# A gated linear-attention recurrence with 64x64 array quarters for its rows, logits and scores

## The chip, the cores and the metric

One core of a Trainium2 chip runs the whole program. The metric is the device time of one execution in microseconds (us): the median of several executions of the same compiled program.

## The reference

The program is three stages in a row; the change touches the first alone. In code, cut to what matters:

```python
# q, k, v, f_logit: [4, 8, 768, 48] = batch, heads, sequence, head size
f = 1 / (1 + exp(-f_logit))
for t in range(768):
    state = f[:, :, t, :, None] * state + einsum('bhd,bhe->bhde', k[:, :, t], v[:, :, t])
    y[:, :, t] = einsum('bhd,bhde->bhe', q[:, :, t], state)
x = y as 3072 rows of 384
logits = (x / |x|) @ (emb / |emb|).T / tau      # 8 experts
out = gate * (relu(x @ w1[e]) @ w2[e])          # e = the best expert of the row
a = out @ m1; b = out @ m2; result = ((a * b) @ w3) @ w_out
```

## The kernel before, in words

The recurrence is computed in 24 tiles of 128 time steps (6 chunks of 4 batches; all 8 heads in each tile). The products of a tile on TensorE are, in the order in which one step s issues them (`step` of the tensor block):

- `scores(s)`: for each head, keys times queries, 48 (stored as 64) rows of contraction, 128x128 out, into the banks `b_a0` and `b_a1`. VectorE's `mask(s)` multiplies them by a triangle and puts them into `am`.
- `cumulate(s+2)`: a triangle of ones times the logarithms of the decay, in two parts (`lg_hi`, `lg_lo`), into `b_cum`. VectorE's `bound` takes the smaller of the sums and 60 into `cc`; ScalarE's `exps` makes exp(-cc) into `ec` and exp(cc) into `en`; GpSimd's `scale_q` multiplies the queries by `ec`, VectorE's `scale_k` the keys by `en`.
- `rows_and_logits(s-1)`: turns the finished y of the tile before (copied by ScalarE's `copy_yT` to `yT`, features on partitions) into rows with time on partitions, by products with `pick`, an identity beside the expert embeddings, into the bank `b_x`. VectorE's `take_rows` copies the rows to `x_ring` and sums the logits over the head pairs.
- `turn_qk(s+1)`: transposes of the scaled queries and keys into `b_qT` and `b_kT`, copied by ScalarE (`copy_qT`) and VectorE (`copy_kT`).
- `state_products(s)`: the carried state times the queries, 64x48 weights, into y's banks `b_y0` and `b_y1`.
- `chunk_products(s)`: values times the masked scores, added to the same banks; then y is done.
- `update_products(s)`: keys times values into `b_up`, a part of y's second bank. VectorE's `carry` adds the state, GpSimd's `decay` multiplies by the last decay of the tile, which goes through DRAM (`save_last`, `load_last` on the SP queue).

Each operation on float32 weights stands as two loads and two matmuls in the trace. Every engine runs its own `step` for s = -3 to 24; what sets the order is this written order on each engine, the semaphores between them and rings of four buffers for the loads. Steps 5 to 20 are a loop; in it ScalarE (`high_w3`, `high_wo`), VectorE (`low_wo`) and GpSimd (`low_w3`) also split two weight matrices into high and low parts, which stage three needs. After the last tile TensorE goes on with products of those weights (`w34_product`) while the rows are sorted by expert, and the two feed-forward stages follow.

An array "quarter" is a weight block on rows 0 to 63 or 64 to 127 and columns 0 to 63 or 64 to 127 of TensorE. Which one an instruction uses follows from the partitions of its operands (rows) and of its output (columns).

Of the kernel before, what the change touches and what calls it, by code (L numbers as in the profile page):

```python
# [27 lines left out]
P = 128  # L28
# [4 lines left out]
HP = 64  # L33
CH = S // P
# [24 lines left out]
CEIL = 60.0  # L59
# [53 lines left out]
def build(nc, ctx, qkvf, emb, tau, sets1, sets2, w3_t, w_out, out):  # L113
# [58 lines left out]
    cc = early("cc", [P, DM])  # L172
# [13 lines left out]
    pick = early("pick", [P, NP, 2 * D + E])  # L186
# [43 lines left out]
    SL = [pick[0:1].rearrange("p j n -> p (j n)")[:, k * (SLOTS + 2) * E:(k + 1) * (SLOTS + 2) * E].rearrange(  # L230
# [44 lines left out]
    YB = NP // 2 * P  # L275
    b_up = b_y1[:, YB:YB + NP * D]
# [4 lines left out]

    def y_place(j, g):

        if j < NP // 2:
            return b_y0[g * HP:g * HP + D, j * P:(j + 1) * P]
        return b_y1[(1 - g) * HP:(1 - g) * HP + D, (j - NP // 2) * P:(j - NP // 2 + 1) * P]
# [21 lines left out]
    clamp_done, ef_done, lg_done, ll_done, cum_done, bound_done, ec_done, exp_done = (sem(n) for n in (  # L308
        "clamp_done", "ef_done", "lg_done", "ll_done", "cum_done", "bound_done", "ec_done",
        "exp_done"))  # L310
# [33 lines left out]
    def _(sp):  # L344
# [60 lines left out]
        sp.wait_ge(pick_done, 1)  # L405
        for h in range(H):
            place = (h % 2 if h // 2 < NP // 2 else 1 - h % 2) * HP
            sp.dma_start(pick[place:place + D, h // 2, 2 * D:],
                         emb[:, h * D:(h + 1) * D].rearrange("e d -> d e"), allow_slow_non_contiguous=True
                         ).then_inc(emb_in, 16)  # L410
# [118 lines left out]
    def _(pool):  # L529
# [88 lines left out]
        pool.wait_ge(clamp_done, 2)  # L618
        pool.memset(ec[:, :, :, D:], 1.0)
# [53 lines left out]
    def _(pe):  # L673
        pe.wait_ge(masks_done, 3)

        def warm(n):

            for _ in range(n):
                pe.transpose(b_x[:, 0:P], ident[:], ident[:])

        def cumulate(i, r):

            pe.wait_ge(ll_done, i + 1)
            need(pe, bound_done, i)
# [18 lines left out]
        def state_products(i, r):  # L703
            for j in (0, NP // 2, 1, NP // 2 + 1):
                for g in range(2):
                    mm = pe.matmul(y_place(j, g), state[g * HP:(g + 1) * HP, r % 4, j, :],  # L706
                                   qT[g * HP:(g + 1) * HP, r % 2, j, :], start=(j % (NP // 2) == 0), stop=False,
                                   skip_group_check=True)
            mm.then_inc(sp_done, 1)

        def update_products(i, r):

            pe.wait_ge(ks_done, i + 1)
# [7 lines left out]
        def chunk_products(i, r):  # L721
            pe.wait_ge(am_done, i + 1)
            pe.wait_ge(v_landed[r % 4], (i - r % 4) * 4 + 16)
            for j in range(NP):
                for g in range(2):
                    h = 2 * j + g
                    mm = pe.matmul(y_place(j, g), ring_v[:, r % 4, h * D:(h + 1) * D],  # L727
                                   am[:, g, j, :], start=False, stop=True, skip_group_check=True)
# [13 lines left out]
        def rows_and_logits(i):  # L742

            pe.wait_ge(yT_done, i + 1)
            need(pe, rl_done, i)
            for j in range(NP):
                mm = pe.matmul(b_x[:, j * (2 * D + E):(j + 1) * (2 * D + E)], yT[:, j * P:(j + 1) * P], pick[:, j, :],  # L747
                               start=True, stop=True)
            if isinstance(i, int) and i == NORM_AT:
                pe.wait_ge(ones_done, 1)  # L750
                pe.wait_ge(en_sq_done, 1)
                mm = pe.matmul(b_x[:, NP * (2 * D + E):NP * (2 * D + 2 * E)], ones[:],
# [860 lines left out]
```

## Time and profile before

| | us |
|---|---|
| median of 3 runs | 716.99 |
| lowest, highest | 716.39, 717.34 |
| the profiled execution | 716.52 |
| its span | 714.6 |
| TensorE busy | 705.7 |
| VectorE, ScalarE, GpSimd busy | 339.8, 292.8, 193.2 |
| granted TensorE clock | 1.0 |

The span runs from the first to the last instruction. The recurrence takes about its first 143 us; the rest is the sorting and the two feed-forward stages. Busy shares are means over all stages, so the stage that is changed has to be read by itself: its timeline, the order of the operations on each engine, and what each waited for.

### The profile page before, as it was taken

The page shows a single profiled execution, that of the slowest core. Times are in us where ns is not written, and L with a number is a line of the kernel's source. Part 1 is how long each engine was busy: PE and PEld are TensorE (multiplying, and loading weights), DVE is VectorE, ACT ScalarE, POOL GpSimd, SP SyncE. Part 2 cuts the span into 40 slices and gives each one's busy share as a digit, 9 for nine tenths or more (in the row PEclk, how much of TensorE's full clock was granted, in tenths as well). Part 3 has the DMA queues.
Part 4 walks back from the last instruction along what each step waited for, and adds up shares of the span by engine and source line. Part 5 has one row for each costly group of instructions (what it writes and reads, how often), then busy time and mean ns, then how long its engine had stood idle before and what let it go on. Part 6 is the DMA issues. An engine that isn't in the chain of part 4 may idle for free.

```text
span 714.6 us, 13946 instructions
## 1 busy us (share of the span) xinstructions
PE 705.7 (99%) x4863; PEld 643.7 (90%) x4863; DVE 339.8 (48%) x564; ACT 292.8 (41%) x559; POOL 193.2 (27%) x197
## 2 busy tenths in 40 slices
PE   7999999999999999999999999999999999999997
PEld 6988888899999999999999988988989989889887
DVE  6888899678753545536556441312212112112121
ACT  5788888534443444435445342123022022121220
POOL 4567777202412022000000013034042051150242
PEclk9999999999999999999999999999999999999999
DMA  7788886261854443524244220000000010000001
GB/s 219 210 234 246 247 247 188 59 188 45 253 150 129 131 132 113 154 85 133 89 132 129 91 89 1 1 22 23 0 33 11 0 44 0 11 33 0 22 22 44
DMA packets 73056, 70.79 MB, mean 99 GB/s; under 512 B 20520, under 2 KB 61480, under 8 KB 73024
## 3 DMA queue, kind: packets, MB, share of 16 engines
q1 hardware_dynamic: 69952, 60.95, 28.9%
q0 software_dynamic: 3072, 9.44, 4.1%
q8 instruction: 17, 0.28, 0.2%
q14 instruction: 15, 0.12, 0.0%
HBM read 60.88 MB, written 9.49 MB: 98 GB/s over the span
## 4 chain that ended last, share of the span: by engine, by line
PE 94%; DVE 2%; issue 1%; DMA 1%; POOL 1%; ACT 1%; POOLq 0%; ACTq 0%; DVEq 0%; SPq 0%
PE b_a L768 10%; PE b_a L770 10%; PE b_a L769 10%; PE bank L768 9%; PE bank L770 9%; PE bank L769 9%; PE b_y L768 6%; PE b_y L769 6%; PE b_y L770 6%; PE b_a L694 4%; PE b_y L727 3%; PE bank L747 3%; PE bank L738 3%; PE b_y L706 2%; PE b_y L717 1%; PE bank L685 1%
## 5 line engine op out<-in xcount | busy, mean ns | idle before, releaser
L653 POOL TENSOR_TENSOR p_lo<-prod,p_hi 128x512 fp32r<-128x512 f32 x42 | 53.9, 1284 | 333.3 <-ACT p_hi L1154 333.3
L1151 ACT COPY a_sb<-b_a 128x512 f32<-128x512 f32 x48 | 28.2, 587 | 218.2 <-PE bank L770 218.2
L1562 DVE TENSOR_TENSOR prod<-bank,a_sb 128x512 f32<-128x512 f32 x48 | 33.2, 692 | 165.7 <-ACT a_sb L1151 165.7
L1104 ACT ACTIVATE h_hi<-b_a 128x432 fp32r<-128x432 f32 x64 | 34.0, 532 | 124.3 <-PE b_a L770 124.0
L1518 DVE SCALAR_TENSOR_TENSOR h_lo<-b_a,h_hi 128x432 fp32r<-128x432 f32 x64 | 38.8, 607 | 96.0 <-ACT h_hi L1104 96.0
L1179 DVE TENSOR_TENSOR w_lo<-w_raw,w_hi 128x768 fp32r<-128x768 f32 x72 | 67.9, 956 | 5.3 <-ACT w_hi L1067 1.2
L770 PE MATMUL b_a<-x_hi,w_lo 128*128 128x432 f32 x192 | 68.7, 358 | 0.0
L769 PE MATMUL b_a<-x_lo,w_hi 128*128 128x432 f32 x192 | 68.7, 358 | 0.0
L768 PE MATMUL b_a<-x_hi,w_hi 128*128 128x432 f32 x192 | 68.7, 358 | 0.0
L1067 ACT CAST w_hi<-w_raw 128x768 fp32r<-128x768 f32 x72 | 58.5, 833 | 0.0
L768 PE MATMUL b_a<-m_hi,w_hi 128*128 128x512 f32 x144 | 56.1, 390 | 0.6 <-DVE w_lo L1179 0.6
L769 PE MATMUL b_a<-m_lo,w_hi 128*128 128x512 f32 x144 | 56.1, 390 | 0.0
L770 PE MATMUL b_a<-m_hi,w_lo 128*128 128x512 f32 x144 | 56.1, 390 | 0.0
L768 PE MATMUL bank<-m_hi,w_hi 128*128 128x512 f32 x144 | 56.0, 389 | 0.0
L769 PE MATMUL bank<-m_lo,w_hi 128*128 128x512 f32 x144 | 56.0, 389 | 0.0
L770 PE MATMUL bank<-m_hi,w_lo 128*128 128x512 f32 x144 | 56.0, 389 | 0.0
L627 POOL DMA_INDIRECT xs<-x_recurrence,ids x24 | 25.9, 1080 | 110.4 <-PE bank L862 76.3
L768 PE MATMUL b_y<-h_hi,w_hi 128*128 128x432 f32 x128 | 46.9, 367 | 0.2
L769 PE MATMUL b_y<-h_lo,w_hi 128*128 128x432 f32 x128 | 45.7, 357 | 0.0
L770 PE MATMUL b_y<-h_hi,w_lo 128*128 128x432 f32 x128 | 45.7, 357 | 0.0
L768 PEld LDWEIGHTS b_a<-x_hi,w_hi 128*128 128x128 f32 x192 | 36.1, 188 | 1.5
L770 PEld LDWEIGHTS b_a<-x_hi,w_lo 128*128 128x128 f32 x192 | 36.1, 188 | 1.4
(247 smaller groups left out, 1626.1 us busy)
## 6 DMA issues: line engine op xcount, KB each, us to landing
w_raw<-sets SPq DMA_DIRECT2D x80, 192.0 KB, 3.5
w_raw<-sets SPq DMA_DIRECT2D x40, 384.0 KB, 4.0
ring_all<-qkvf SPq DMA_DIRECT2D x24, 384.0 KB, 3.8
ring_fc<-qkvf SPq DMA_DIRECT2D x24, 192.0 KB, 3.7
ring_all<-qkvf SPq DMA_DIRECT2D x24, 192.0 KB, 3.0
x_recurrence<-x_all SPq DMA_DIRECT2D x24, 192.0 KB, 3.6
w_sb<-w_t SPq DMA_DIRECT2D x8, 512.0 KB, 4.6
wo_sb<-w_out SPq DMA_DIRECT2D x8, 192.0 KB, 4.2
```

Source lines behind the costliest of these rows:

```text
L627: pool.indirect_dma_start(out=xs[:, w % BATCH, :], out_offset=None, in_=rec_dram.rearrange("b c p n -> (b c p) n"), in_offset=bass.Indirec ...
L653: pool.tensor_tensor(p_lo[:, f, :], prod[:, f % 2, :], p_hi[:, f, :].bitcast(F32), ALU.subtract).then_inc(pl_done, 1)
L694: mm = pe.matmul([b_a0, b_a1][g][:, j * P:(j + 1) * P], kT[g * HP:(g + 1) * HP, r % 2, j, :], qT[g * HP:(g + 1) * HP, r % 2, j, :], start= ...
L768: pe.matmul(acc, a_hi, b_hi, start=first, stop=False, skip_group_check=skip)
L769: pe.matmul(acc, a_hi, b_lo, start=False, stop=False, skip_group_check=skip)
L770: return pe.matmul(acc, a_lo, b_hi, start=False, stop=last, skip_group_check=skip)
L1067: act.copy(piece(w_hi, f), piece(w_raw, f)).then_inc(wh_done, 1)
L1104: act.activation(h_hi[:, f % 2, 0:SW], b_h[f % 2][:, 0:SW], ACT.Relu).then_inc(hh_done, 1)
L1151: act.copy(a_sb[:, f % 2, :], b_a[f % 2][:]).then_inc(as_done, 1)
L1179: return dve.tensor_tensor(out_, whole, high.bitcast(F32), ALU.subtract)
L1518: dve.scalar_tensor_tensor(out=h_lo[:, f % 2, 0:SW], in0=b_h[f % 2][:, 0:SW], scalar=0.0, in1=h_hi[:, f % 2, 0:SW].bitcast(F32), op0=ALU.m ...
L1562: dve.tensor_tensor(prod[:, f % 2, :], b_b[f % 2][:], a_sb[:, f % 2, :], ALU.mult).then_inc(pr_done, 1)
```

## The change

- Scores: each 64x128 weight block becomes two 64x64 blocks, so 16 products in place of 8, in the order in which four neighbours use the four quarters.
- Rows and logits: `yT` is laid out so that heads 0 to 3 stand on partitions 0 to 47 and heads 4 to 7 on 64 to 111 (`y_place`). The 4 products of 128x128 weights with 104 columns become 16 products of 48x64 weights with 56 columns, in quarters. They go to the inner halves of y's two banks (`b_rows`).
- The update gets `b_x`, the bank that rows had; `copy_yT` no longer waits for `carry` to have read it.
- `bound` is taken out. `exps` reads `b_cum` itself, and `scale_k` takes the smaller of `en` and exp(60) in the same instruction that multiplies the keys.
- Order on TensorE: `rows_and_logits` directly behind `scores`, then `cumulate`. On VectorE: `take_rows` ahead of `mask`; `mask` in two instructions, and `chunk_products` waits for each half; `low_logs` always behind `copy_kT`. On ScalarE: `copy_yT` ahead of `high_w3`.
- New waits: `state_products` waits for `rl_done` (VectorE has read the rows out of y's banks). `quarter()` issues an increment of a semaphore that nobody waits for, three times per tile on TensorE's queue. `exps(0)` waits for the padding of `ec`, which GpSimd writes later than before.
- At the start a memset of `yT` and two of four copies for `pick` go; the numbers of filling matmuls change from 14, 0, 10 to 16, 0, 4.

```diff
+    NS = NP // 2
+    y_parts = y_all.rearrange("p (a n) -> p a n", n=YB)[:, 0:4:3, :]
+    b_rows = y_all[:, 512 - NP * (D + E):512 + NP * (D + E)].rearrange("p (k n) -> p k n", n=D + E)
+    b_up = b_x[:, 0:NP * D]
     def y_place(j, g):
+        c = j // NS
+        return b_y01[c * HP:c * HP + D, g, g * YB + j % NS * P:g * YB + (j % NS + 1) * P]
...
+        def quarter():
+            pe.sem_inc(quarters, 1)
         def cumulate(i, r):
             pe.wait_ge(ll_done, i + 1)
-            need(pe, bound_done, i)
+            need(pe, exp_done, i)
         def scores(i, r):
             pe.wait_ge(qT_done, i + 1)
             pe.wait_ge(kT_done, i + 1)
-            need(pe, am_done, i)
+            need(pe, am_done, 2 * i)
+            quarter()
             for j in range(NP):
                 for g in range(2):
-                    mm = pe.matmul([b_a0, b_a1][g][:, j * P:(j + 1) * P], kT[g * HP:(g + 1) * HP, r % 2, j, :],
-                                   qT[g * HP:(g + 1) * HP, r % 2, j, :], start=True, stop=True)
+                    for c in range(2):
+                        mm = pe.matmul([b_a0, b_a1][g][c * HP:(c + 1) * HP, j * P:(j + 1) * P],
+                                       kT[g * HP:(g + 1) * HP, r % 2, j, c * HP:(c + 1) * HP],
+                                       qT[g * HP:(g + 1) * HP, r % 2, j, :], start=True, stop=True)
-        def state_ready(i):
-            need(pe, yT_done, i)
-            need(pe, sum_done, min(i, NT - B) if isinstance(i, int) else i)
-            need(pe, s_done, i - B + 1)
         def state_products(i, r):
+            need(pe, s_done, i - B + 1)
+            need(pe, rl_done, i)
+            quarter()
         def update_products(i, r):
-            pe.wait_ge(ks_done, i + 1)
+            need(pe, sum_done, min(i, NT - B) if isinstance(i, int) else i)
         def chunk_products(i, r):
-            pe.wait_ge(am_done, i + 1)
             pe.wait_ge(v_landed[r % 4], (i - r % 4) * 4 + 16)
+            for j in range(NS):
+                pe.wait_ge(am_done, 2 * i + (j + 1))
         def rows_and_logits(i):
             pe.wait_ge(yT_done, i + 1)
-            need(pe, rl_done, i)
-            for j in range(NP):
-                mm = pe.matmul(b_x[:, j * (2 * D + E):(j + 1) * (2 * D + E)], yT[:, j * P:(j + 1) * P], pick[:, j, :],
-                               start=True, stop=True)
+            quarter()
+            for j in range(NS):
+                for g in range(2):
+                    for c in range(2):
+                        for t in range(2):
+                            cols = slice((g * NS + j) * P + t * HP, (g * NS + j) * P + (t + 1) * HP)
+                            mm = pe.matmul(b_rows[t * HP:(t + 1) * HP, c * NP + 2 * j + g, :],
+                                           yT[c * HP:c * HP + D, cols], pick[c * HP:c * HP + D, 2 * j + g, :],
+                                           start=True, stop=True)
...
         def exps(i, r):
-            act.wait_ge(bound_done, i + 1)
+            act.wait_ge(cum_done, i + 1)
+            if isinstance(i, int) and i == 0:
+                act.wait_ge(pads_done, 2)
         def copy_yT(i):
             act.wait_ge(y_done, i + 1)
-            if not isinstance(i, int) or i < NT - B:
-                act.wait_ge(sum_done, i + 1)
...
         def scale_k(i, r):
-            dve.tensor_tensor(ks[:, r % 2, :, 0:D], ring_qk[:, r % 4, DM:2 * DM].rearrange("p (h d) -> p h d", h=H),
-                              en[:, r % 2, :].rearrange("p (h d) -> p h d", h=H), ALU.mult).then_inc(ks_done, 1)
-        def bound(i):
-            dve.wait_ge(cum_done, i + 1)
-            need(dve, exp_done, i)
-            dve.tensor_scalar_min(cc[:], b_cum[:, 0:DM], CEIL).then_inc(bound_done, 1)
+            dve.scalar_tensor_tensor(out=ks[:, r % 2, :, 0:D], in0=en[:, r % 2, :].rearrange("p (h d) -> p h d", h=H),
+                                     scalar=TOP,
+                                     in1=ring_qk[:, r % 4, DM:2 * DM].rearrange("p (h d) -> p h d", h=H),
+                                     op0=ALU.min, op1=ALU.mult).then_inc(ks_done, 1)
         def mask(i):
+            for j in range(NS):
+                dve.tensor_tensor(am[:].rearrange("p g (c j) t -> p g c j t", c=2)[:, :, :, j, :],
+                                  b_a01.rearrange("p g (c j t) -> p g c j t", c=2, t=P)[:, :, :, j, :],
+                                  upto[:].unsqueeze(1).unsqueeze(1).to_broadcast([P, 2, 2, P]), ALU.mult
+                                  ).then_inc(am_done, 1)
```

## Rows read from the trace of the kernel before

**Rows 1.** Windows: busy us (x) of PE, PEld, DVE, ACT, POOL; clock; DMA share; GB/s.

```profile
71.00:82.00 11.00, 11.00 (x176) 9.77 (x169) 10.09 (x20) 9.53 (x23) 8.39 (x9) 1.00 0.87 255
```

**Rows 2.** TensorE's timeline over one tile: start, duration, operation, count.

```profile
24.84 1.03 PE L747 MATMUL bank<-pick,yT 128*128 128x104 f32 x8
25.71 0.60 PE L738 MATMUL bank<-ident,qs 128*128 128x128 f32 x4
...
26.67 0.65 PE L706 MATMUL b_y<-qT,state 64*48 64x128 f32 x16
27.26 1.08 PE L727 MATMUL b_y<-am,ring_all 128*48 128x128 f32 x16
28.17 0.62 PE L717 MATMUL b_y<-ring_all,ks 128*64 128x48 f32 x16
28.72 1.16 PE L694 MATMUL b_a<-qT,kT 64*128 64x128 f32 x16
29.81 0.45 PE L685 MATMUL bank<-lg_hi,upto_r 128*128 128x384 f32 x1
```

**Rows 3.** TensorE's timeline: the scores of tiles 1 and 20.

```profile
17.86 1.16 PE L694 MATMUL b_a<-qT,kT 64*128 64x128 f32 x16
...
122.04 1.16 PE L694 MATMUL b_a<-qT,kT 64*128 64x128 f32 x16
```

**Rows 4.** Duration of one matmul in ns (min/median/max), by source line.

```profile
L706 PE MATMUL b_y<-qT,state x31: 269/269/307, 87.1 to 93.0; 64*48 64x128 f32 x31
...
L717 PE MATMUL b_y<-ring_all,ks x16: 206/222/222, 88.6 to 89.0; 128*64 128x48 f32 x16
```

**Rows 5.** VectorE's timeline in one tile.

```profile
89.88 0.55 DVE L1194 TENSOR_TENSOR ks<-ring_all,en 128x384 f32<-128x384 f32 x1
90.37 1.23 DVE L1210 TENSOR_TENSOR am<-b_a,upto 128x1024 f32<-128x1024 f32 x1
91.51 0.55 DVE L1200 TENSOR_SCALAR cc<-bank 128x384 f32<-128x384 f32 x1
92.05 0.89 DVE L1184 TENSOR_TENSOR lg_lo<-lg,lg_hi 128x384 fp32r<-128x384 f32 x1
92.86 0.55 DVE L1229 COPY x_all<-bank 128x384 f32<-128x384 f32 x1
...
93.43 0.68 DVE L1205 COPY kT<-bank 128x512 f32<-128x512 f32 x1
```

**Rows 6.** ScalarE's timeline in the same tile, with the idle time in brackets.

```profile
88.90 0.62 ACT L1015 CAST w_hi<-w_sb  x1
90.03 0.59 ACT L1000 COPY yT<-b_y 128x512 f32<-128x512 f32 x1 [0.51 <-issue]
```

**Rows 7.** GpSimd's and SP's timeline in the same tile.

```profile
90.78 1.28 POOL L577 TENSOR_TENSOR w_lo<-w_sb,w_hi  x1 [1.30 <-DVE ks L1194]
92.01 0.51 POOL L567 TENSOR_TENSOR state<-s_sum,e_all 128x192 f32<-128x192 f32 x1
...
93.29 0.39 SPq L370 DMA_DIRECT2D e_all<-last_rows  x1
```

**Rows 8.** The page's DMA issues: count, KB each, median us to landing.

```profile
e_all<-last_rows SPq DMA_DIRECT2D x24, 2.0 KB, 2.5
```

**Rows 9.** ScalarE's copy of y in the tile of rows 2 (timeline).

```profile
23.84 0.59 ACT L1000 COPY yT<-b_y 128x512 f32<-128x512 f32 x1 [1.12 <-PE b_y L727]
```

**Rows 10.** TensorE's sequencer instructions behind it: ns each, first and last start.

```profile
L72 PEldq EVENT_SEMAPHORE  x2: 51/51/51, 24.5 to 24.6; - x2
...
L736 PEldq EVENT_SEMAPHORE  x1: 51/51/51, 24.7 to 24.7; - x1
```

**Rows 11.** The first exponentials of the program, on ScalarE (timeline).

```profile
7.85 0.52 ACT L984 ACTIVATE ec<-cc 128x384 f32<-128x384 f32 x1 [1.33 <-DVE cc L1200]
```

**Rows 12.** TensorE's timeline in the last tile: rows, then state products.

```profile
138.84 1.06 PE L747 MATMUL bank<-pick,yT 128*128 128x104 f32 x8
139.83 0.65 PE L706 MATMUL b_y<-qT,state 64*48 64x128 f32 x16
```

More of the change, by code:

```diff
@@ L58 @@
 FLOOR = -40.0
-CEIL = 60.0
+TOP = float(np.exp(60.0))
 LEAST = 39.0
@@ L185, in build @@
     x_tile = early("x_tile", [P, DM])
-    pick = early("pick", [P, NP, 2 * D + E])
+    pick_all = early("pick_all", [P, NP * (2 * D + E)])
+    pick = pick_all[:, 0:NP * (D + E)].rearrange("p (k n) -> p k n", k=NP)
     upto = early("upto", [P, P])
@@ L229, in build @@
         "p (v i) -> p v i", v=3)
-    SL = [pick[0:1].rearrange("p j n -> p (j n)")[:, k * (SLOTS + 2) * E:(k + 1) * (SLOTS + 2) * E].rearrange(
+    SL = [pick_all[0:1, k * (SLOTS + 2) * E:(k + 1) * (SLOTS + 2) * E].rearrange(
         "p (t e) -> p t e", e=E) for k in range(2)]
@@ L404, in _ @@
         load_v(RING - 1, RING - 1)
-        sp.wait_ge(pick_done, 1)
+        sp.wait_ge(pick_done, 2)
         for h in range(H):
-            place = (h % 2 if h // 2 < NP // 2 else 1 - h % 2) * HP
-            sp.dma_start(pick[place:place + D, h // 2, 2 * D:],
+            place = h // NP * HP
+            sp.dma_start(pick[place:place + D, h % NP, D:],
                          emb[:, h * D:(h + 1) * D].rearrange("e d -> d e"), allow_slow_non_contiguous=True
@@ L721, in chunk_products @@
         def chunk_products(i, r):
-            pe.wait_ge(am_done, i + 1)
             pe.wait_ge(v_landed[r % 4], (i - r % 4) * 4 + 16)
-            for j in range(NP):
+            for j in range(NS):
+                pe.wait_ge(am_done, 2 * i + (j + 1))
                 for g in range(2):
-                    h = 2 * j + g
-                    mm = pe.matmul(y_place(j, g), ring_v[:, r % 4, h * D:(h + 1) * D],
-                                   am[:, g, j, :], start=False, stop=True, skip_group_check=True)
+                    for n in (j, j + NS):
+                        h = 2 * n + g
+                        mm = pe.matmul(y_place(n, g), ring_v[:, r % 4, h * D:(h + 1) * D],
+                                       am[:, g, n, :], start=False, stop=True, skip_group_check=True)
             mm.then_inc(y_done, 1)
@@ L751, in rows_and_logits @@
                 pe.wait_ge(en_sq_done, 1)
-                mm = pe.matmul(b_x[:, NP * (2 * D + E):NP * (2 * D + 2 * E)], ones[:],
-                               en_sq[:].rearrange("p j e -> p (j e)"), start=True, stop=True)
+                mm = pe.matmul(b_norm, ones[:], en_sq[:].rearrange("p j e -> p (j e)"), start=True, stop=True)
             mm.then_inc(xl_at, 1)
@@ L786, in step @@
             if isinstance(s, int) and s < 0:
-                warm({-3: 14, -2: 0, -1: 10}[s])
+                warm({-3: 16, -2: 0, -1: 4}[s])
             if (i := tile_of(s, 0)) is not None:
                 scores(i, r)
-            if (i := tile_of(s, 2)) is not None:
-                cumulate(i, r + 2)
             if isinstance(s, int) and s == NT:
@@ L802, in step @@
                 rows_and_logits(i)
-            if (i := tile_of(s, 0)) is not None:
-                state_ready(i)
+            if (i := tile_of(s, 2)) is not None:
+                cumulate(i, r + 2)
             if (i := tile_of(s, 1)) is not None:
@@ L1017, in step @@
         def step(s, r, part=None):
+            if (i := tile_of(s, -1)) is not None:
+                copy_yT(i)
             if part:
                 high_w3(*part)
-            if (i := tile_of(s, -1)) is not None:
-                copy_yT(i)
             if (i := tile_of(s, 3, 2)) is not None:
@@ L1251, in step @@
                 scale_k(i, r + 1)
-            if (i := tile_of(s, 0)) is not None:
-                mask(i)
-            if (i := tile_of(s, 2)) is not None:
-                bound(i)
-            if early_logs(s) and (i := tile_of(s, 3, 1)) is not None:
-                low_logs(i, r + 3)
             if isinstance(s, int) and s == NT:
@@ L1261, in step @@
                 take_rows(i, (r + RING - 1) % RING)
+            if (i := tile_of(s, 0)) is not None:
+                mask(i)
             if isinstance(s, int) and s == -3:
@@ L1265, in step @@
                 dve.wait_ge(emb_in, 16 * H)
-                dve.tensor_tensor(en_sq[:], pick[:, :, 2 * D:], pick[:, :, 2 * D:], ALU.mult).then_inc(en_sq_done, 1)
+                dve.tensor_tensor(en_sq[:], pick[:, :, D:], pick[:, :, D:], ALU.mult).then_inc(en_sq_done, 1)
             if (i := tile_of(s, 1)) is not None:
                 copy_kT(i, r + 1)
-            if not early_logs(s) and (i := tile_of(s, 3, 1)) is not None:
+            if (i := tile_of(s, 3, 1)) is not None:
                 low_logs(i, r + 3)
```

77 lines of the change are left out of this document (30 added, 47 removed).

## The prediction

> **What bounds the kernel now.** I read the windows first: in the steady recurrence TensorE is busy for 11.00 of 11.00 us at full granted clock, VectorE for 10.09, ScalarE for 9.53, GpSimd for 8.39, and the DMA engines are 0.87 busy [rows 1]. So this stage ends as fast as TensorE gets through its list, but the others follow closely, and a shorter list helps only as far as they can follow. Next I read TensorE's timeline. It has no gap: each group starts where the one before leaves off [rows 2]. From scores to scores it would be 5.43 us (the 3.88 us from 24.84 to 28.72, plus 1.09 us of scores and 0.46 us of `cumulate` up to the next rows). From tile 1 to tile 20 the scores take 104.18 us for 19 steps, 5.48 us each [rows 3]; the 0.05 us more is a wait for `yT`, whose copy ends at 90.62 us [rows 6] and which I take to be just too late for the rows there.
>
> In these groups several small products run side by side. A timeline row's duration less that of one matmul is the time from its first to its last start [rows 2, 4]:
> - state products, 16 matmuls on four quarters: 0.65 - 0.27 = 0.38 us, so about 0.11 us for each wave of four once it runs. Transposes of the same 128 columns come 0.11 us apart ((0.60 - 0.27) / 3), so a wave costs what one lone matmul does.
> - update, 16 matmuls with 64-column weights, two side by side: 0.62 - 0.22 = 0.40 us, so 0.057 us a wave. The whole array is loaded anew in each.
> - rows, 8 matmuls of the full array: 0.87 us to the next group, 0.109 us each.
> - between groups that cut the array differently nothing starts for some time: state to chunk 0.59 - 0.38 = 0.21 us, update to scores 0.55 - 0.40 = 0.15 us.
>
> **Part by part, TensorE.** *Scores.* Eight waves of two halves become eight of four quarters, with the same columns to stream. Before, they take 1.09 us with the change of cut behind them. After, by the state products: 0.38 us for the first four waves, 0.44 us for four more, 0.11 us to the next group, 0.93 us. *Rows.* 32 matmuls in eight waves, 56 columns in place of 104. The nearest row for short columns on newly loaded 64-column weights is the update: 0.057 us a wave, 0.40 us in all, 0.02 us for the last two starts, and 0.15 us for the change of cut to `cumulate`: 0.57 us. *Sum.* Scores and rows with their cuts cost 1.09 + 0.87 = 1.96 us before and 0.93 + 0.57 = 1.50 us after: 0.46 us less. The number of changes of cut per tile stays at four. From 5.43 us this gives 4.97 us a tile. Chunk and update keep their products; state keeps its eight in another order, still four quarters per wave.
>
> Rows' wave has bounds. It cannot beat the update's 0.057 us, since it loads as much; if the loads of one half's two quarters go one after the other it is about 0.11 us, and rows last as long as before. I take the lower end, because the update shows two loads of 64 columns side by side in different columns, and the scores of today two in different rows.
>
> *The sequencer.* Three increments per tile are added and two waits more on `am`. One of its own instructions takes 51 ns [rows 10]. They are hidden while matmuls are queued behind which it runs ahead; with the waits for rows, `cumulate` and `turn_qk` now behind shorter groups, some may show. Bounds: nothing, or all of four to six of them, 0.2 to 0.3 us a tile. I take 0.08 us, near the lower end, as the same kind of wait costs nothing visible today [rows 2].
>
> **The other engines at 4.97 us a tile.** I walk one tile, with T = 0 at the first scores matmul. *VectorE* [rows 5]: removing `bound` frees 0.54 us (91.51 to 92.05). The mask takes 1.14 us for 1024 columns; two halves at 0.07 us of fixed cost each make 1.20 us. `scale_k` has the same 384 columns and keeps its 0.55 us (bounds: no less, and 0.3 us more if the two-step form ran at a slower rate; the idle time covers it). Rows start at 0.93 us and the last ends at 0.93 + 0.42 + 0.22 = 1.57 us, so `take_rows` runs from 1.6 to 2.2 us, the mask's halves end near 2.9 and 3.5 us, `copy_kT` at 4.1 us. Against that, TensorE: `cumulate` from 1.5 us, transposes 1.95 to 2.9 us, state from 2.9 us (it needs the rows read: 2.2), chunk from 3.5 us (first half of the mask: 2.9; second half needed at 4.0, there at 3.5), next scores at 4.97 us (`kT`: 4.1). The new wait for `rl_done` thus has 0.7 us to spare; behind it state, chunk and update are queued. VectorE's busy 10.09 of 11 us is 5.0 us a tile, 4.5 us after. *ScalarE* [rows 6]: 9.53 of 11 us is 4.75 us a tile, of which nothing goes, so 0.2 us is left. Its copy of y now starts when y is done rather than behind `carry`: 0.6 us earlier than rows need it, which ends the 0.05 us wait. The exponentials read the bank itself at no higher price that I can name: copies of 512 columns from banks take 0.59 us, the cast from the other memory 0.62. *GpSimd* waits 1.30 us for `ks` [rows 7] and has room. *SP and DMA*: the state's last decay goes round through DRAM: decay starts at 92.01, `e_all` is asked for at 93.29 [rows 7], lands 2.5 us later [rows 8]: 3.8 us, under 4.97. DMA would be 0.87 x 5.48 / 4.97 = 0.96 busy, which is near its end; but the rings are four tiles deep.
>
> **Start and end.** The first exponentials start at 7.85 us behind `bound` [rows 11]. Without it they start 0.56 us earlier, and `low_logs(0)`, now ahead of the copies for `pick`, 0.5 us earlier still; the chain to the first scores shifts by both, unless the slower clock of the first us holds the transposes back: 1.0 us, bounds 0.5 and 1.2. At the end, the last tile's state products follow rows after 0.99 us [rows 12]; now they wait for `take_rows` too: 0.57 us of rows, 0.2 us of a cut, 0.7 us of VectorE, so 0.5 us is lost.
>
> **Sum.** 19 steps x (5.48 - 4.97) = 9.7; three further steps (0, 20, 21 and 22 in part) 1.4; start 1.0; end -0.5; sequencer 21 x -0.08 = -1.7: 9.9 us. Behind the recurrence TensorE stays busy and what is sorted there depends on the last rows, so all of it moves forward together. The profiled execution took 716.52 us, 0.47 us under the median; 716.52 - 9.9 = 706.6, and I give 706.5 as the median (the 0.47 is within the spread of the three runs).
>
> **Rivals.**
> *A, the forecast*, own range 703 to 709.5.
> *B, the quarters do not make rows shorter.* No group of the trace starts matmuls closer than 0.38/15 = 25 ns apart on the mean (update 27 ns). If the one or the other is a floor for starts, rows take 32 x 25 or 27 ns = 0.80 or 0.87 us in place of 0.47 to the next group; 23 x 0.33 or 0.40 = 7.6 or 9.2 us of the gain is gone: 714 or 715.7, what remains being start, scores and the `yT` wait. Loads in turn give the latter. For it: no row has a shorter mean. Against it: state and update are each fully explained by columns and loads. The Trainium skill, "TensorE: Matmul & The Clock Gate", section "Wait — 56ns, not 53.3ns?", says that start-to-start does not fall below about 25 ns however few the columns; by that the time would be about 714. No row here decides it, as none has four short products side by side.
> *C, slower: TensorE's instructions come too slowly.* A tile has 164 loads and matmuls before, 244 after. State and update use 32 each in 0.55 to 0.59 us, 17 to 18 ns apiece. If that were the supply's rate, 244 would take 4.2 us, and some 15 sequencer instructions at 0.1 us each by their spacing [rows 10] another 1.5: 5.75 us a tile, 0.27 us over today, 22 x 0.27 = +6: 722. It is slower than before from 16 ns apiece. Against: between the end of `yT`'s copy at 24.43 us [rows 9] and the sequencer instruction at 24.7 [rows 10] lie the 16 loads and matmuls of rows and two of its own, 0.17 / 16 = 11 ns each at most.
> *D, another engine takes over.* ScalarE has 0.2 us to spare and DMA 4%; if either holds the tile at 5.15 to 5.25 us, 22 x 0.2 to 0.3 is lost: 710 to 712.
>
> **How the numbers follow.** A 0.62, B 0.16, C 0.06, D 0.16. Range: A and D whole, and up to B's cheaper end: 702.5 to 714, which leaves out C, most of B and little of A's lower side. Faster by over 0.2% (1.4 us, about what can be told from no change) are A, D and nearly all of B: 0.92; within it 0.03 of B; slower C and a little more: 0.05.
>
> **What would show it.** Scores to scores near 5.05 us; rows' 32 matmuls about 0.64 us long in the timeline (0.42 + 0.22; over 1.0 under B); `cumulate` 1.5 us behind the scores' start; no idle time on TensorE beyond the cuts; VectorE idle before `take_rows`. Gaps in both load and matmul rows inside scores and rows would speak for C, idle time of TensorE put down to ScalarE, VectorE or a DMA for D. The prediction is wrong if a tile takes over 5.35 us or under 4.9.

## The result and the profile after

The changed kernel takes 712.06 us in the median (709.97 to 714.45), the kernel before 716.57 us (715.37 to 717.34) in the same rounds: a ratio of 0.994, 95% interval 0.9922 to 0.9957. That is 4.5 us less, where about 10 were forecast. The profiled execution took 709.99 us, its span is 708.2 us.

The span and the chain of work that ended last, on the page of the changed kernel:

```profile
span 708.2 us, 15892 instructions
...
PE 84%; DMA 5%; issue 4%; POOL 2%; DVE 2%; SPq 2%; ACT 1%; POOLq 0%; ACTq 0%; DVEq 0%
```

The chain holds 5% of DMA (4% is `e_all<-last_rows`), in the kernel before 1%. Something that used to be hidden now ends waits. The windows say where (changed kernel; columns as in [rows 1]; the first stretch is most of the loop, the other two lie inside it):

```profile
45.00:112.00 67.00, 64.34 (x1546) 56.30 (x1548) 57.66 (x115) 58.49 (x141) 52.63 (x52) 1.00 0.87 255
42.00:53.00 11.00, 11.00 (x278) 9.96 (x278) 10.14 (x21) 10.09 (x25) 7.61 (x8) 1.00 0.84 235
97.00:108.00 11.00, 10.18 (x244) 8.88 (x244) 8.86 (x19) 9.37 (x23) 8.23 (x10) 1.00 0.86 249
```

TensorE is busy without a gap early in the loop, as in [rows 1], but lacks 2.66 us of the 67. What a tile costs it shows in its timeline. The first of these two tiles runs through, the second waits:

```profile
79.07 1.10 PE L705 MATMUL b_a<-qT,kT 64*64 64x128 f32 x32
79.97 0.67 PE L763 MATMUL b_y<-pick_all,yT 48*64 48x56 f32 x32
...
81.02 0.60 PE L750 MATMUL bank<-ident,qs 128*128 128x128 f32 x4
...
81.98 0.65 PE L717 MATMUL b_y<-qT,state 64*48 64x128 f32 x16
82.57 1.08 PE L739 MATMUL b_y<-am,ring_all 128*48 128x128 f32 x16
83.48 0.62 PE L728 MATMUL bank<-ring_all,ks 128*64 128x48 f32 x16
84.03 1.10 PE L705 MATMUL b_a<-qT,kT 64*64 64x128 f32 x32
84.95 0.64 PE L763 MATMUL b_y<-pick_all,yT 48*64 48x56 f32 x32
85.52 0.44 PE L694 MATMUL bank<-lg_hi,upto_r 128*128 128x384 f32 x1
...
86.47 0.63 PE L750 MATMUL bank<-ident,qs 128*128 128x128 f32 x4 [0.33 <-POOL qs L564]
```

Scores (L705) to scores is 84.03 - 79.07 = 4.96 us, against 5.43 us in [rows 2]. Scores take 0.92 us to rows (84.95 - 84.03), rows (L763) 0.57 us to `cumulate` (85.52 - 84.95). So the products became as short as forecast. The wait is for the scaled queries, behind GpSimd. From tile 8 on it comes in every second tile: the scores start 4.96 us apart in one and 5.47 to 6.00 us in the next; ahead of it the long ones take up to 5.18 us. The mean from tile 3 to tile 20 is 5.21 us.

Who waited for what from 40 to 110 us (changed kernel; us in total, times, longest). The kernel before has no wait for `e_all` in this stretch:

```profile
POOL state L572 <- DMA e_all<-last_rows: 9.3, 8, 2.0
POOL w_lo L582 <- DVE ks L1206: 7.6, 8, 1.6
DVE x_all L1238 <- PE b_y L763: 5.0, 10, 0.7
PEld bank L750 <- POOL qs L564: 4.4, 6, 1.1
...
PE bank L750 <- POOL qs L564: 2.7, 6, 0.8
```

GpSimd's `decay` (L572) waits for the decay row that goes through DRAM, and `turn_qk` (L750) waits for the queries that GpSimd scales afterwards. The round can be followed in the timelines of GpSimd and of SP's queue (changed kernel, two of the views put one after the other):

```profile
77.04 0.51 POOL L572 TENSOR_TENSOR state<-s_sum,e_all 128x192 f32<-128x192 f32 x1
...
83.50 0.60 POOL L572 TENSOR_TENSOR state<-s_sum,e_all 128x192 f32<-128x192 f32 x1 [1.58 <-DMA e_all<-last_rows]
84.08 1.27 POOL L558 TENSOR_SCALAR ring_fc<-ring_fc 128x384 f32<-128x384 f32 x1
85.31 1.01 POOL L564 TENSOR_TENSOR qs<-ring_all,ec 128x384 f32<-128x384 f32 x1
...
94.60 0.51 POOL L572 TENSOR_TENSOR state<-s_sum,e_all 128x192 f32<-128x192 f32 x1 [1.81 <-DMA e_all<-last_rows]
```

```profile
76.02 0.34 SPq L352 DMA_DIRECT2D ring_fc<-qkvf  x1
76.61 0.36 SPq L382 DMA_DIRECT2D x_recurrence<-x_all  x1
77.19 0.35 SPq L395 DMA_DIRECT2D w_sb<-w_t  x1
77.77 0.34 SPq L364 DMA_DIRECT2D ring_all<-qkvf  x1
78.39 0.39 SPq L375 DMA_DIRECT2D e_all<-last_rows  x1
...
84.36 0.34 SPq L364 DMA_DIRECT2D ring_all<-qkvf  x1
85.10 0.39 SPq L375 DMA_DIRECT2D e_all<-last_rows  x1
...
88.85 0.34 SPq L364 DMA_DIRECT2D ring_all<-qkvf  x1
89.38 0.39 SPq L375 DMA_DIRECT2D e_all<-last_rows  x1
```

By the code `decay` of one tile (77.04) frees the buffer for which `load_v` waits on SP; behind `load_v` (77.77) the next `e_all` is asked for (78.39), and the next `decay` needs it. This load took 4.9 us, landed at 83.29, and `decay` began at 83.50: 6.5 us from `decay` to `decay`. The next load was asked for at 85.10 and landed after 2.4 us, in time: 4.25 us (to 87.75). The alternation is one round over two tiles. In the long half SP doesn't wait for `decay` at all: that of 77.04 ended at 77.55, and SP issued without a pause up to 78.39. The same holds for the loads asked for at 68.49, 89.38 and 99.87 us; ahead of those at 47.06 and 57.69 us SP still waited, by 0.2 to 0.6 us. What makes that request late is SP's own list since its last pause, so the wait that counts is the one before. After `decay` at 83.50 SP is released (`load_v` at 84.36), issues a whole stage without a pause (next `load_v` at 88.85, 4.5 us), asks for `e_all` at 89.38, waits 4.9 us for the landing, and `decay` begins at 94.60. That is 11.1 us for two tiles, where TensorE's list needs 9.9. From issue to landing of the loads asked for at 78.39 and 85.10:

```profile
DMA to landing us min/median/max: 4.9/4.9/4.9
...
DMA to landing us min/median/max: 2.4/2.4/2.4
```

All of them from 53 to 107 us in turn: 2.7, 4.7, 2.6, 4.1, 2.1, 4.9, 2.4, 4.9, 2.4, 5.1, 2.3 us. In the kernel before the same loads took 2.5, 3.1, 2.3, 3.6, 2.6, 2.8, 2.3, 3.5, 2.5, 3.1 us: the median of [rows 8] hides that every second one is slower. The load of [rows 7] itself, asked for at 93.29 us, is the one of 3.5 us. The long ones are those that SP issues without a pause behind its other transfers (a new one every 0.6 us from 76.02 on, in the rows above); ahead of a short one it had paused (from 74 us on its `load_v` came 2.5 to 3.2 us behind the transfer before).

The time to each point of TensorE's timeline, summed as the forecast summed it (us gained on the kernel before, profiled executions):

| stretch | forecast | measured |
|---|---|---|
| up to the scores of tile 2 | 1.0 + 2 x 0.43 = 1.9 | 23.29 - 22.39 = 0.9 |
| 18 steps, tiles 2 to 20 | 18 x 0.43 = 7.7 | 98.75 - 93.78 = 5.0 |
| tiles 20 to 23 | 0.8 | 15.08 - 13.78 = 1.3 |
| last tile, to the products behind its rows | -0.5 | 6.38 - 7.12 = -0.7 |
| sum | 9.9 | 143.50 - 137.07 = 6.4 |

(0.43 us is the forecast's 5.48 - 4.97 less its 0.08 for the sequencer; 0.8 is what then remains of its sum.) Two places lost it: the loop by 2.7 us and the start by 1.0 us; tiles 20 to 23 gained 0.5 us more than forecast. The profiled executions are 6.5 us apart and the medians 4.5; on these 2 us more below.

At the start a different wait shows. GpSimd, SP and TensorE in tile 1 of the changed kernel (timelines):

```profile
17.07 1.17 POOL L558 TENSOR_SCALAR ring_fc<-ring_fc 128x384 f32<-128x384 f32 x1 [4.52 <-DMA ring_fc<-qkvf]
...
6.87 6.99 SPq L413 DMA_DIRECT2D pick_all<-emb  x8
13.91 0.47 SPq L352 DMA_DIRECT2D ring_fc<-qkvf  x1
...
19.35 0.63 PE L750 MATMUL bank<-ident,qs 128*128 128x128 f32 x4 [1.24 <-POOL qs L564]
```

Scores of tile 1 came at 15.77 us, 2.1 us earlier than in [rows 3]. But the decay logits of tile 4 are asked for behind eight loads of the expert embeddings, which hold SP's queue for 7 us, and the clamp of tile 4 stands ahead of the next scaled queries on GpSimd. Tile 1 takes 6.62 us, and 0.9 us is left.

### The profile page after: what moved, and what is told of

It reads as the page before. It is cut to its first block, busy times and chain, and to the rows that moved or that the text cites. A ratio compares the mean times of both kernels' runs of the same rounds, so it can differ in the third digit from the quotient of the medians.

```text
span 708.2 us, 15892 instructions
## 1 busy us (share of the span) xinstructions
PE 694.9 (98%) x5819; PEld 632.1 (89%) x5819; DVE 330.3 (47%) x562; ACT 291.6 (41%) x559; POOL 191.6 (27%) x197
## 4 chain that ended last, share of the span: by engine, by line
PE 84%; DMA 5%; issue 4%; POOL 2%; DVE 2%; SPq 2%; ACT 1%; POOLq 0%; ACTq 0%; DVEq 0%
PE b_a L784 10%; PE b_a L786 10%; PE b_a L785 10%; PE bank L784 9%; PE bank L786 9%; PE bank L785 9%; PE b_y L784 6%; PE b_y L786 6%; PE b_y L785 6%; DMA e_all<-last_rows 4%; PE b_y L739 1%; PE b_a L705 1%; PE bank L750 1%; PE bank L876 1%; PE b_y L717 1%
## 5 line engine op out<-in xcount | busy, mean ns | idle before, releaser
L785 PEld LDWEIGHTS b_a<-x_lo,w_hi 128*128 128x128 f32 x192 | 36.2, 188 | 1.5
```

Of the source, the lines that this page charges most:

```text
L785: pe.matmul(acc, a_hi, b_lo, start=False, stop=False, skip_group_check=skip)
```

## The experiments

The theory after this reading: in the loop the round through DRAM (`decay`, SP's wait ahead of `load_v`, SP's list, `e_all`, `decay`) holds the tile, and at the start the load of tile 4's logits; the products themselves do what was forecast. The rivals: the lost time belongs to TensorE's own list (waits for the mask's halves, more instructions to fetch), with the wait for `e_all` only in its shadow; the round is long because of one 512 KB weight load ahead of it, not because of its place behind a wait; or a part of the gain is not the array's at all but that of `bound`. All times are medians with the range; each ratio is against the kernel before on the same chip, whose medians were 716.45, 716.56 and 716.51 us.

**The round cut.** `e_all` is asked for one step of the queue earlier, ahead of the wait that follows the last `decay`; all transfers stay.

```diff
+        load_last(1, 1)
         def stage(m, u):
             i = m * RING + u
             load_v(i, u)
-            load_last(i - 3, (u + 1) % RING)
             save_last(i - 2, (u + 2) % RING)
             load_qk(i + 1, (u + 1) % RING)
             load_f(i + 3, (u + 3) % RING)
             store_x(m - 1, u)
+            load_last(i - 2, (u + 2) % RING)
...
```

> The changed kernel with the load of e_all moved from behind load_v (which waits for decay) to the end of SP's stage before, ahead of the weight load. Theory R (the tile is held by a round: decay, load_v's wait, e_all issued behind it, landing, next decay): the 15.0 us that GpSimd waits for e_all go to under 2, scores to scores of tiles 3 to 20 is 4.95 to 5.0 us in place of 5.28, and the time falls 4 to 6 us below the changed kernel, to 706 to 708. Theory S (the DMA engines are simply full at this pace, 0.82 to 0.88 busy): landings get no shorter, other loads come late in their place, and the time stays within 1.5 us of the changed kernel's 712.1.

Measured: 709.36 us (706.68 to 711.15), ratio 0.9898 (0.9868 to 0.9928), 2.7 us below the changed kernel where theory R expected 4 to 6; the waits for `e_all` went as it said, and over tiles 3 to 20 a tile takes 5.07 us, one pause among them (6.32 us for tile 5), where 4.95 to 5.0 was expected. Repeated beside the changed kernel itself, with nothing new in either:

> r1_round_cut unaltered, on the same chip. The round's worth is the difference to a0_again: 2.7 us by the medians so far, 4 by the steady tiles of the two profiles ((5.21 - 4.98) x 17). I expect 708 to 710, 2.5 to 4 us under a0_again.

> The changed kernel unaltered, to stand beside the three others on one chip and to see a second profile, since its first profile was its quickest execution but one (709.99 against a median of 712.06). If its ordinary executions lose their 2 us in the round too, a profile near 712 shows over 15 us of waits of GpSimd for e_all and steady tiles of 5.3 us; if they lose it at the start, tiles 1 to 5 take over 27 us in place of 26.4.

Measured: 708.18 us (707.19 to 710.49) with the round cut, 712.95 us (709.48 to 714.92) without. On one chip the cut is worth 4.8 us; by the ratios of the first runs (0.994 and 0.9898) 3.0 us. The executions of the changed kernel spread over more than this (5.4 us), so 3 to 5 us is as near as the runs say. The repeated kernel's windows and its waits of the longest kind from 40 to 110 us:

```profile
45.00:112.00 67.00, 67.00 (x1620) 59.95 (x1622) 62.19 (x122) 62.39 (x150) 52.98 (x55) 1.00 0.87 263
...
POOL w_lo L582 <- DVE ks L1206: 17.4, 15, 2.7
...
POOL state L572 <- DMA e_all<-last_rows: 0.7, 2, 0.4
```

TensorE has no gap left in this window; from 48.36 to 113.01 us thirteen steps take 4.973 us each. The changed kernel, taken again, waited 11.9 us for `e_all` in that stretch. The loads have not become quicker: with the round cut they land after 2.7 to 5.0 us, 3.8 in the median. They are just no longer behind the wait on `decay`. That refutes the rival of TensorE's own list: it is the same list, and it takes 4.97 us a tile.

**The weight load moved, the round kept.** `load_w3` goes from the end of the stage to behind `save_last`, so that it doesn't stand directly ahead of `load_v` and `e_all`.

```diff
             load_last(i - 3, (u + 1) % RING)
             save_last(i - 2, (u + 2) % RING)
+            if weights:
+                load_w3(m, u // 2, u % 2)
...
-                load_w3(m, u // 2, u % 2)
```

> The changed kernel with the weight load (512 or 192 KB) moved within SP's stage to directly behind save_last, so that e_all is no longer the next load behind it but four later; the round through decay stays. Theory R with its second half (e_all lands in 4.9 us when it is issued right behind the 512 KB load and in 2.1 us otherwise): the largest landing of e_all falls from 5.1 to under 3.5 us, GpSimd waits for e_all under 3 us in all, the time is 706.5 to 709. Theory S: landing max stays above 4.5 us and the time within 1.5 us of 712.1.

Measured: 710.11 us (709.14 to 710.51), ratio 0.9907 (0.989 to 0.9924). The long tiles stay (scores 5.05, 4.97 and 6.70 us apart around 60 us), with the wait, and every second landing is long still, 4.0 to 5.8 us, the 4.0 with the weight load asked for 3 us ahead:

```profile
POOL state L573 <- DMA e_all<-last_rows: 9.3, 10, 3.0
```

So it isn't the one transfer directly ahead, and this half of the theory of the weight load falls. By its ratio it may have gained some 2 us on the changed kernel all the same; its profile, with the same wait, doesn't show where.

**The same cut in the kernel before.** Same edit, on the kernel with 5.43 us of products.

> The same move of the e_all load as in r1, made in the kernel before. Theory R: there TensorE's own 5.43 us per tile is longer than the round, so the time moves by less than 1 us (at most the 4.5 us that GpSimd waits at two places at the start become shorter without TensorE noticing). Theory S: also no move. A gain of 3 us or more would say that the round already held the kernel before and the comparison of the two kernels has to be read anew.

Measured: 716.35 us (715.15 to 716.9), ratio 0.9995 (0.9986 to 1.0005). The round costs nothing at the old pace; it came in as the new limit only with shorter products.

**`bound` alone.** Only this part of the change, on the kernel before: the sums read from the bank, the clamp in `scale_k`.

```diff
-            act.wait_ge(bound_done, i + 1)
+            act.wait_ge(cum_done, i + 1)
...
-            dve.tensor_tensor(ks[...], ring_qk[...], en[...], ALU.mult)
+            dve.scalar_tensor_tensor(out=ks[...], in0=en[...], scalar=float(np.exp(60.0)),
+                                     in1=ring_qk[...], op0=ALU.min, op1=ALU.mult)
```

> The kernel before with one part of the change alone: bound taken out, exps reads the sums from their bank, the smaller of en and exp(60) is taken inside scale_k. My forecast's terms: 0.5 us at the start (the first exponentials at about 7.3 us) and 0.05 us or less per tile: 715.0 to 716.2 against 716.6. Rival: VectorE, not TensorE, was what held the last hundredths of a tile, and the time falls by 2 us or more. Rival: reading the bank costs ScalarE more and the time rises by 1 us or more.

Measured: 716.08 us (715.01 to 716.76), ratio 0.9997 (0.9987 to 1.0007). Nothing that can be told. Its tiles take 5.46 us (19 steps from 17.83 to 121.63 us) against 5.48: VectorE had time to spare at that pace, as [rows 1] shows. That doesn't say that `bound` could have stayed: by the prediction VectorE would be busy for 5.0 us a tile with it, against a list of 4.97 us on TensorE. The changed kernel with `bound` put back was not run.

**The start.** Tile 4's and 5's logits ahead of the embeddings, once with the round cut and once on the changed kernel alone.

```diff
         load_v(RING - 1, RING - 1)
+        load_f(RING, 0)
+        load_f(RING + 1, 1)
         sp.wait_ge(pick_done, 2)
         for h in range(H):
             ...
-        load_f(RING, 0)
         save_last(0, 0)
-        load_f(RING + 1, 1)
```

> The changed kernel with e_all out of the round (as in r1) and, at the start, the loads of f for tiles 4 and 5 ahead of the eight slow loads of the expert embeddings on SP's queue. In r1 scores of tile 1 to scores of tile 2 took 8.7 us, TensorE idle 1.7 us for qs behind a late f and then at half clock for some 3 us. Theory (what is left is this start): scores 1 to 2 falls to 5.0 to 5.8 us, scores 1 to 20 to 95 to 97 us, and the time is 703.5 to 706. Rival: the embeddings, now 0.9 us later, hold the first rows instead and it stays at 707 or more.

> The changed kernel with the start's loads moved alone, the round left. If the start and the round are separate losses, scores 1 to 2 falls from 6.6 to 5.0 to 5.8 us and the time by 1 to 1.7 us to 710.5 to 711; tiles 3 to 20 stay at 5.2 to 5.3 us. If the round takes it back (being ahead earlier only lengthens the waits for e_all), the time stays at 712.

Measured: 708.6 us (707.66 to 710.96) with both, ratio 0.9904; 711.97 us (711.13 to 712.85) with the start alone, ratio 0.9944. Both came as their rivals said: 707 us or more, and no gain with the round left. Moving the two loads shows no gain over the round cut alone (709.36 and 708.18 us). Tile 1 fell from 6.62 to 5.83 and 6.07 us, but its rows then wait for the last embedding (0.64 and 0.88 us). With the start alone, scores(20) came at 117.13 us, where the changed kernel has 116.17 and 116.44: the long tiles (up to 6.4 us) took back all that the start had given. With one of the two loads moved:

> r1 with one load of f (tile 4) ahead of the embeddings, in place of the two of s2_both, where the first rows waited 0.64 us for the embeddings. If that trade is what is left at the start, scores 1 to 2 takes 5.0 to 5.6 us and the time is 0.3 to 1 us under s2_both, 707.5 to 708.5; if f of tile 5 is then late, tile 2 takes over 5.5 us and nothing is gained over s2_both.

Measured: 707.27 us (705.03 to 707.78), ratio 0.9874 (0.9854 to 0.9893), the lowest median of all and clear of both kernels. Against the round cut alone on the same chip (708.18 us, 707.19 to 710.49) it is 0.9 us less, with ranges that overlap: what the start is worth is not shown beyond its profile. TensorE's timeline in tile 1 and its window over the loop:

```profile
15.60 1.10 PE L705 MATMUL b_a<-qT,kT 64*64 64x128 f32 x32
17.16 0.69 PE L763 MATMUL b_y<-pick_all,yT 48*64 48x56 f32 x32 [0.46 <-DMA pick_all<-emb]
...
21.24 1.10 PE L705 MATMUL b_a<-qT,kT 64*64 64x128 f32 x32
...
45.00:112.00 67.00, 67.00 (x1655) 60.30 (x1654) 61.71 (x122) 62.22 (x150) 53.24 (x55) 1.00 0.90 267
```

Its profiled execution took 705.03 us, 4.96 less than the changed kernel's, and the places add up to it within 0.1 us: 1.15 us at the scores of tile 2 (22.39 - 21.24) and 93.78 - 89.92 = 3.86 us over the next 18 steps, now 5.00 us each.

**The scores alone.** The old scores (64x128 weights, half the products), with start and round mended and on the changed kernel.

```diff
-                    for c in range(2):
-                        mm = pe.matmul([b_a0, b_a1][g][c * HP:(c + 1) * HP, j * P:(j + 1) * P],
-                                       kT[g * HP:(g + 1) * HP, r % 2, j, c * HP:(c + 1) * HP], ...)
+                    mm = pe.matmul([b_a0, b_a1][g][:, j * P:(j + 1) * P], kT[g * HP:(g + 1) * HP, r % 2, j, :], ...)
```

> As s2_both, but with the scores in eight 64x128 products as before the change. TensorE then is the bound in all steady tiles, so the scores' quarters show their worth there: before they took 1.09 us with the cut behind them, now 0.93 us to the rows; 24 x 0.16 = 3.8 us slower than s2_both.

> The changed kernel with the old scores alone, round and start left. If the round of decay and e_all holds most tiles, a longer TensorE list is largely hidden: 0.5 to 2 us slower than the changed kernel, under half of what s2_old_scores loses against s2_both. If TensorE held the tiles after all, it loses the same 3.8 us.

Measured: 710.38 us (709.57 to 716.56) and 713.29 us (712.58 to 713.75), 1.8 us over their like with quarters (708.6) and 1.2 us over the changed kernel in its first rounds (0.3 us over its repetition). The forecast of 3.8 us for the first was missed, the second lies at the low end of 0.5 to 2. The median of the first hides two kinds of execution: six took 709.6 to 710.5 us, four took 715.2 to 716.6 us, with a mean granted clock of 0.995 to 0.998 against 0.999 to 1.0. The profiled one is of the quick kind; where the others lose 5 to 6 us is not shown. One of its tiles, mended start and round, on TensorE:

```profile
84.49 1.16 PE L704 MATMUL b_a<-qT,kT 64*128 64x128 f32 x16
85.58 0.69 PE L761 MATMUL b_y<-pick_all,yT 48*64 48x56 f32 x32
86.20 0.45 PE L694 MATMUL bank<-lg_hi,upto_r 128*128 128x384 f32 x1
...
89.67 1.16 PE L704 MATMUL b_a<-qT,kT 64*128 64x128 f32 x16
```

The tile takes 5.18 us: 1.09 us for scores in place of 0.92, and 0.62 us for rows in place of 0.57. The quarters in the scores are thus worth 0.22 us a tile, 0.17 of it in the scores themselves. Over 20 tiles that would be 4.4 us, and the medians show less. Where the round isn't cut, part is explained: 5.37 us a tile over tiles 2 to 20 against 5.21 to 5.26, as the round over two tiles is the limit either way. With it cut, single pauses (below) cost the profiled execution with quarters about 2 us (tiles 3 and 7 took 6.70 and 5.59 us) that the one without them didn't have; whether that is so in the others is not known.

**Fewer bytes ahead of the round.** On the changed kernel, from tile 4 on the values' loads bring 16 of 384 columns (this leaves out part of `v`; the products on it remain).

> The changed kernel with the round left, but the loads of v from tile 4 on bring 16 of 384 columns, so that the output of the recurrence is wrong from tile 4 on and 0.18 MB less per tile are moved, the load right ahead of e_all among them. Every instruction and wait is the same. Theory Q (e_all lands late because it queues behind what SP has just issued): its largest landing in the steady tiles falls from 5.1 to under 4.2 us, GpSimd waits under 4 us for it in tiles 5 to 20, and the time is 707 to 710. Theory L (the landing has a length of its own, whatever is queued): landings and the time stay as in a0_again.

Measured: 709.94 us (708.2 to 710.34), 3.0 us under the changed kernel on the same chip (709.48 to 714.92). The wait for `e_all` from 40 to 110 us falls to 3.9 us from 11.9, and the alternation ends at tile 12:

```profile
POOL state L573 <- DMA e_all<-last_rows: 3.9, 4, 1.7
```

The order on SP's queue and its waits are unchanged here, so bytes that are under way when the small load is asked for lengthen its landing: from 45 us on it took 2.7 us in the median. Whether those ahead of it on its queue do this or the load on all DMA engines, whose busy share fell from 0.86 to 0.77 too, the run doesn't separate. The slowest still took 4.9 us, against the under 4.2 us expected, so they aren't all of it.

## Why the prediction was right and wrong

- *The list of TensorE: right.* Scores 0.92 us (0.93 forecast), rows 0.57 us (0.57), a tile 4.96 us (4.97). The rows' 32 products last 0.64 us in the timeline, as said. Rival B is refuted: less its last one (218 ns) that is 0.42 us for 31 starts, 14 ns from one to the next on the mean. The Trainium skill, "TensorE: Matmul & The Clock Gate", section "Wait — 56ns, not 53.3ns?", would have it at 25 ns or more; with small weights in four quarters the trace doesn't agree, and the measurement decides. The kernel before had no such group, so its rows could not settle it.
- *The sequencer: its 0.08 us a tile was too much.* Tiles that wait for nothing take 4.96 us, so all the added increments and waits are hidden; 1.7 us of the forecast's sum was not needed. C is refuted with it for the steady tiles; single pauses stay open, see below.
- *The waits: right.* `state_products` behind `rl_done` shows no wait in a tile that runs through, the 0.05 us for `yT` is gone. `scale_k` takes 0.59 us in the median rather than 0.55, but up to 1.40 us, beyond the bound of 0.3 us more. TensorE's waits in the loop are put down to the queries, not to it.
- *Start: wrong in both parts.* The first exponentials start at 6.75 us, 1.1 us earlier as worked out, but the first scores came 1.8 us earlier (11.26 against 13.09 us), over the bound of 1.2. What is late next was not asked: the load of tile 4's logits. It took back 1.2 us of the 2.1 us that tile 1 was ahead, and the step missed 1.0 us.
- *End: right*, -0.65 us of the -0.7 is state behind rows (133.34 - 131.70 = 1.64 us against 0.99 in [rows 12]), and -0.5 was forecast.
- *SP and DMA: the step that failed.* "3.8 us, under 4.97" took one round with the median landing [rows 7, 8]. Three things were wrong in it. The median stood for two kinds of landing, of which the slow one took up to 3.6 us from 53 us on (4.1 us for one asked for at 49.33): the tile of [rows 7] itself made 4.8 us, not 3.8. Nothing was allowed for the quicker pace, at which SP issues one transfer behind another and the slow kind takes 4.1 to 5.1 us; from `decay` to `decay` that is 1.35 us to the request, 4.9 us to the landing and 0.2 us: 6.5 us in place of 3.8. And SP's own list was left out, 4.5 us for a stage: at this pace SP is still busy with it when `decay` is done, so the round closes over two tiles, 11.1 us in place of 9.9. That `clamp` and `scale_q`, 2.3 us of GpSimd, stand between a late `decay` and `turn_qk` was not asked either. Over tiles 3 to 20 the mean is 5.21 us. The busy share was not the limit: 0.96 was worked out for the new pace, and it is 0.87 with the round as it was and 0.87 and 0.90 at 4.97 and 5.00 us a tile. The forecast said "the rings are four tiles deep", but this load is in no ring of that depth: it is asked for behind a wait on the `decay` of the tile before.
- *The rivals.* D came true in its number, 5.15 to 5.25 us a tile; measured 5.21 us. Its reason is not what the runs show: it had DMA at the end of its throughput, and what holds the tile is the time of one small load and the order around it. So that agreement is in part luck, and its chance was 0.16. Its sum was off as well: 22 x 0.2 to 0.3 is 4.4 to 6.6 us, from 706.5 that gives 710.9 to 713.1, not 710 to 712. A, with 0.62, described the loop of the kernel with its round cut, 4.97 us a tile; that kernel's two medians are 709.36 and 708.18 us, in A's range and 2.9 and 1.7 us above its 706.5.

The Trainium skill, "DMA: Bandwidth & Descriptors", section "Queues, rings and completion order", says that each DMA engine takes the descriptors of a ring in their order. The run with few columns of `v` is in line with it (wait for `e_all` 3.9 us in place of 11.9): with fewer bytes issued ahead of it on its queue a load of 2 KB lands earlier. It doesn't prove it, since all DMA engines had less to do as well.

*What stays open.* The medians of the changed kernel and of its repetition lie 2 to 3 us above their profiled executions. The repetition was to show such an ordinary execution, but its profile is a quick one again (710.2 us). Stalls of TensorE have a second price in one profile: in the first run with the round cut tile 1 waited 1.73 us for the queries, and the granted clock fell (columns as in [rows 1]; then TensorE's timeline). Its 0.66 is a mean over a stretch at both levels, 2.4 and 1.2 GHz:

```profile
19.00:24.00 5.00, 4.29 (x50) 3.60 (x51) 2.35 (x3) 2.98 (x9) 3.17 (x4) 0.66 0.66 147
...
19.71 0.63 PE L750 MATMUL bank<-ident,qs 128*128 128x128 f32 x4 [1.73 <-POOL qs L564]
...
22.07 1.86 PE L739 MATMUL b_y<-am,ring_all 128*48 128x128 f32 x16
```

The chunk products took 1.86 us, which take 1.08 at full clock, and this tile 8.72 us in place of 6.6. But the length of the wait alone doesn't decide it. With 1.24 us the changed kernel kept its clock, and so did the run with few columns of `v` with 1.98 us at the same place (19.62 us):

```profile
19.00:24.00 5.00, 4.38 (x119) 4.01 (x120) 2.61 (x5) 4.43 (x12) 3.69 (x6) 1.00 0.39 91
```

What the runs do show of the difference: where the clock fell, TensorE had also started the rows of that tile 0.24 us late (16.75 - 15.59 = 1.16 us behind the scores, where 0.92 is usual). That this decides is not shown. Executions of the changed kernel's repetition with a mean clock of 0.995 to 0.998 took 714.0 to 714.9 us, those at 0.999 to 1.0 took 709.5 to 713.7. That the clock falls at this place in those too is argued, not shown; the four long executions with the old scores have such a mean clock as well, and their profiled one has no wait in tile 1. The other open point: four of the profiles with quarters in the rows (three with quarters in the scores too) have a pause of TensorE of 1.0 to 1.7 us between 30 and 44 us that nothing in the trace releases:

```profile
31.56 1.08 PE L739 MATMUL b_y<-am,ring_all 128*48 128x128 f32 x16 [1.66 <-issue]
```

(from the kernel with round and start changed). From 26 to 36 us two 16 KB transfers of the instruction queue fall in this profile; the page counts 21 of them after and 17 before. The kernel of the lowest median has one from 29 to 32.5 us too, without such a pause, so nearness alone proves nothing. The quarters add 80 loads and matmuls to a tile; that their supply makes the pauses was not tried.

Nor is the gain taken apart in full: the quarters in the rows alone, the order of the operations alone, and the change with `bound` left in were not run.

## What to carry to other kernels

When a change shortens the list of the engine that sets the pace, follow every round that goes through DRAM and comes back to itself, once per step or once in two, add all of its parts, the time in which the issuing queue works through its own list among them, and compare it with the new pace and not the old; take the landings one by one, since a median hides a slow kind that comes in every second step, and expect them to be slower at the quicker pace. On a queue, ask for what a round needs ahead of the wait on that same round: here it gave 3 to 5 us, and nothing at the old pace. And an engine that starts earlier needs its next inputs earlier too, so look at what the queue issues behind the first ones.

## What the runs showed of the hardware

- Products of 48x64 weights and 56 columns in four quarters of the array start 14 ns apart on the mean ((0.64 - 0.218) / 31), half of the closest that the kernel before shows (25 ns, state products).
- A load of 2 KB from DRAM landed after 2.1 to 5.8 us. From 74 to 107 us of the changed kernel it took 4.9 to 5.1 us where its queue had issued without a pause, and 2.1 to 2.4 us behind a pause of the queue.
- SP issued its transfers 0.5 to 0.7 us apart when it waited for nothing (76.02 to 78.39 us of the changed kernel: 2.37 us for four steps).
- The rows' products in quarters take 0.62 us to the next group behind scores in halves of the array, and 0.57 us behind scores in quarters.
- Behind a stall of TensorE of 1.73 us, ended at 19.71 us, the granted clock of the stretch was 0.66; around one of 1.24 us at the same place, one of 1.41 us and one of 1.98 us, it stayed at 1.00.
